# Attention and a mixture on one core: keys scaled where they are copied, and four operations moved to other engines or places

## What is computed

```python
k_sum = k.reshape(B, H, nb, block, D).max(axis=3)
v_sum = v.reshape(B, H, nb, block, D).mean(axis=3)
scores_l = scale * np.matmul(q, k.transpose(0, 1, 3, 2))     # scale = 1 / sqrt(64)
scores_s = scale * np.einsum('bhsd,bhnd->bhsn', q, k_sum) + np.log(block)
scores_l_m = np.where(mask_l, scores_l, -1000000000.0)       # |pos - pos'| < 16
a = softmax(concatenate([scores_l_m, scores_s]))
out = np.matmul(a, np.concatenate([v, v_sum], axis=2))
```

```python
logits = x @ w_gate                       # top 2 of 4, softmax over the two
q, k, v = x @ wq[e], x @ wk[e], x @ wv[e]
ye = causal_softmax(q @ k.T / 8) @ v @ wo[e]
```

## Time and profile before

| | |
|---|---|
| median of 3 runs | 451.85 us (450.61 to 452.22) |
| the profiled execution | 452.24 us, its span 450.4 us |
| TensorE busy | 431.9 us, 96% |
| VectorE, ACT, GpSimd busy | 298.1, 227.6, 134.7 us |
| chain that ended last | PE 85%, DVE 8%, ACT 3%, "issue" 3% |
| DMA | 38.12 MB, mean 85 GB/s |

### The profile page before, as it was taken

The page is one execution under the profiler, slowest core; times in us unless marked ns, Lnnn a source line. Parts: engine busy times, 40 slices in busy tenths (PEclk is TensorE's granted clock), DMA queues, the critical chain, the costliest instruction groups (busy, mean ns, idle before and its releaser), DMA issues.

```text
span 450.4 us, 8603 instructions
## 1 busy us (share of the span) xinstructions
PE 431.9 (96%) x3332; PEld 367.1 (81%) x3332; DVE 298.1 (66%) x549; ACT 227.6 (51%) x591; POOL 134.7 (30%) x170
## 2 busy tenths in 40 slices
PE   8799998998997999999999999999999999999997
PEld 3478996887765789978876899998998898989885
DVE  4794489866467835697666877576675776475453
ACT  6785647766237955677782562434443233233120
POOL 3878583000006412000259056631132022200000
PEclk9989998999999999999999999999999999999999
DMA  8965065000493140000022111122123063201103
GB/s 255 261 190 162 26 179 207 1 2 0 123 287 102 25 142 1 0 1 1 1 95 95 47 48 46 49 93 57 46 87 93 0 235 93 72 24 48 47 2 140
DMA packets 13914, 38.12 MB, mean 85 GB/s; under 512 B 1536, under 2 KB 2480, under 8 KB 13872
## 3 DMA queue, kind: packets, MB, share of 16 engines
q1 hardware_dynamic: 13008, 35.98, 26.2%
q10 hardware_dynamic: 864, 1.57, 0.9%
HBM read 31.99 MB, written 4.72 MB: 81 GB/s over the span
## 4 chain that ended last, share of the span: by engine, by line
PE 85%; DVE 8%; ACT 3%; issue 3%; POOL 0%; ACTq 0%; DVEq 0%; POOLq 0%
PE ps_s L683 34%; PE ps_o L683 19%; PE ps_x L683 14%; PE ps_t L683 10%; PE ps_t L855 4%; PE ps_t L750 2%; ACT PA L1094 2%; DVE nmaxM L1443 1%; DVE nmaxA L1351 1%; PE ps_x L869 1%; DVE QS L1391 0%; DVE PTA L1371 0%; DVE PTM L1454 0%; DVE gate_gt L1423 0%; PE ps_s L936 0%
## 5 line engine op out<-in xcount | busy, mean ns | idle before, releaser
L1331 ACT ACTIVATE HID_h<-HID_raw 128x384 fp32r<-128x384 f32 x48 | 25.1, 525 | 72.3 <-DVE HID_raw L1659 31.3
L632 POOL TENSOR_TENSOR W_raw<-W_raw 128x256 f32<-128x256 f32 x11 | 10.7, 975 | 99.3 <-DMA W_raw<-in_ch 88.6
L1094 ACT ACTIVATE PA<-ps_s,biasA 128x120 f32<-128x120 f32 x96 | 33.7, 381 | 12.7 <-DVE biasA L1355 10.1
L683 PE MATMUL ps_s<-C_h,HID_l 128*128 128x512 f32 x96 | 37.7, 393 | 0.0
L683 PE MATMUL ps_s<-C_l,HID_h 128*128 128x512 f32 x96 | 37.7, 393 | 0.0
L683 PE MATMUL ps_s<-C_h,HID_h 128*128 128x512 f32 x96 | 37.6, 392 | 0.0
L547 POOL TENSOR_TENSOR PA<-PA,denA 128x480 f32<-128x480 f32 x24 | 23.7, 986 | 46.7 <-DVE denA L1364 46.6
L1648 DVE SCALAR_TENSOR_TENSOR HID_l<-HID_raw,HID_h 128x384 fp32r<-128x384 f32 x48 | 28.3, 593 | 10.5 <-ACT HID_h L1331 8.1
L1157 ACT ACTIVATE PM<-ps_s,nmaxM 128x128 f32<-128x128 f32 (+5 forms) x48 | 30.1, 634 | 9.5 <-DVE nmaxM L1443 9.0
L683 PE MATMUL ps_o<-V_h,W_h 128*128 128x384 f32 x96 | 32.8, 342 | 0.1
L683 PE MATMUL ps_o<-V_h,W_l 128*128 128x384 f32 x96 | 32.4, 337 | 0.0
(11 more groups left out here) (255 smaller groups left out, 1269.1 us busy)
## 6 DMA issues: line engine op xcount, KB each, us to landing
W_raw<-in_ch SPq DMA_DIRECT2D x12, 512.0 KB, 3.8
C_raw<-in_ch SPq DMA_DIRECT2D x12, 512.0 KB, 3.8
VW<-in_vw SPq DMA_DIRECT2D x12, 384.0 KB, 9.6
KP<-in_kT SPq DMA_DIRECT2D x8, 384.0 KB, 6.4
VT<-in_vT SPq DMA_DIRECT2D x8, 384.0 KB, 6.4
out_x<-US SPq DMA_DIRECT2D x12, 256.0 KB, 2.0
QT<-in_qT SPq DMA_DIRECT2D x7, 384.0 KB, 7.7
raw<-in_tok SPq DMA_DIRECT2D x4, 384.0 KB, 3.3
```

Source lines behind the costliest of these rows:

```text
L632: pool.tensor_tensor(W[S3], W[A11], W[A21], ALU.subtract).then_inc(w_sum, 1)
L683: return pe.matmul(out, lhsT, rhs, start=start, stop=stop)
L1094: last = act.activation(PA[:, u % NPA, j, :], ps_s[u % 2][:, j % 2, (j // 2) * KC:(j // 2 + 1) * KC], ACT.Exp, bias=biasA[:, u % 4, j:j + ...
L1331: act.activation(*own(s, n, half), ACT.Relu).then_inc(g_hi, 1)
```

## The change

Six things, of which the diff below shows the core.

1. `KW` gets the keys and the maxima times 1/8: ACT's copies take a scale, the other copies become multiplications by a constant (TENSOR_SCALAR on GpSimd and VectorE). The masks and logarithms are no longer raised, the exponentials have no scale, and `nmaxA` is their bias as it is: VectorE's scaling to `biasA` and its semaphore are gone, 24 instructions and as many waits.
2. GpSimd makes the splits of wo and of the first half of tok1 ahead of `no_lows` instead of behind it (N_EARLY = 5), and the last split (second half of tok2) waits for the gate's twelfth step.
3. The six stores of u are issued by SP, behind the loads for batch 1, instead of by ACT; the first means' placing stands between the fourth and the fifth store.
4. In batch 0, TensorE makes the first transposes ahead of the first means, and ACT copies in that order.
5. VectorE's fourth sum of the second weight block stands behind X_l instead of ahead of it.
6. With `biasA` gone, the buffers behind it lie 64 bytes lower.

```diff
+N_EARLY = 5
@@ sync
+            def store_u(b, t):
+                sp.wait_ge(m_u, b * TQ + (t + 1))
+                sp.dma_start(u_d[t * P:(t + 1) * P, :], US1[t][:, :]).then_inc(st_u[t], 16)
...
-                for q in range(2):
-                    place_means(b, q)
+                for t in range(TQ):
+                    if t == TQ - 2:
+                        place_means(b, 0)
+                    store_u(b - 1, t)
+                place_means(b, 1)
@@ gpsimd
-                    pool.tensor_copy(KW[:, r, 4 * i:4 * i + 4, 0:WK], windows(r, 4 * i)).then_inc(a_kwin, 1)
+                    pool.tensor_scalar(KW[:, r, 4 * i:4 * i + 4, 0:WK], windows(r, 4 * i), SCALE, None,
+                                       ALU.mult).then_inc(a_kwin, 1)
...
                 if b == 0:
-                    pool.wait_ge(c_lo, 3)
+                    pool.wait_ge(c_lo, N_EARLY)
...
                 if b == 0:
-                    split(len(PACED))
+                    for n in range(len(PACED), N_EARLY):
+                        split(n)
                 no_lows(b)
                 if b == 0:
-                    for n in range(len(PACED) + 1, N_TOK2):
+                    for n in range(N_EARLY, N_TOK2):
+                        if n == N_TOK2 - 1:
+
+                            pool.wait_ge(m_g, NGATE)
                         split(n)
@@ tensor, sequence
+
+                    if k <= NU + 2:
+                        a_transpose(b, k - 3)
                     if b == 0 and k == 3:
                         a_first_means(b)
-
-                    if k <= NU + 2:
-                        a_transpose(b, k - 3)
@@ scalar
-                                          ACT.Exp, bias=biasA[:, u % 4, j:j + 1], scale=SCALE,
+                                          ACT.Exp, bias=nmaxA[:, u % 4, j:j + 1],
...
-                    act.activation(KW[:, r, 4 * i:4 * i + 4, 0:WK], windows(r, 4 * i), ACT.Copy).then_inc(a_kwin0, 1)
+                    act.activation(KW[:, r, 4 * i:4 * i + 4, 0:WK], windows(r, 4 * i), ACT.Copy,
+                                   scale=SCALE).then_inc(a_kwin0, 1)
...
                 for t in range(TQ):
-                    if more:
-                        store_u(b, t)
@@ vector
-                                      AX.X, ALU.max, negate=True).then_inc(a_mx, 1)
-                    dve.wait_ge(a_mx, b * NU + (u + 1))
-                    dve.tensor_scalar(biasA[:, u % 4, :], nmaxA[:, u % 4, :], SCALE, None, ALU.mult).then_inc(a_max, 1)
+                                      AX.X, ALU.max, negate=True).then_inc(a_max, 1)
...
                 m_x2_lo(b, TQ - 1)
+                if not more:
+                    last_row_sum()
```

More of the change, by code:

```diff
@@ L24 @@
 NEG = -1000000000.0
-RAISE = 1.0 / SCALE
 TQ = S // P
@@ L306, in program @@
         a_zero = sem("a_zero")
-        a_mx = sem("a_mx")
         a_kfill0 = sem("a_kfill0"); a_kfill = sem("a_kfill")
@@ L516, in _ @@
             step(pool.memset(mask_m[0:HALF, :, 0:WK], 0.0))
[L517 to L520 removed]
+            keep(mask_m[0:HALF, :, 0:WK], [[0, 3], [1, WK]], -1, -1, NEG)
+            keep(mask_m[0:HALF, :, 0:WK], [[0, 3], [-1, WK]], 2 * WINDOW - 1, 1, NEG)
+            keep(mask_m[0:HALF, 0, 0:WK], [[1, WK]], -WINDOW, 0, NEG)
+            keep(mask_m[0:HALF, 2, 0:WK], [[-1, WK]], WK - WINDOW - 1, 0, NEG)
             assert steps[0] == N_MASK
@@ L1522, in second_row_sums, with last_row_sum @@
                 dve.tensor_tensor(W[S2], W[S1], W[A11], ALU.subtract).then_inc(w_sum1, 1)
+            def last_row_sum():
+                W = [W_raw[1][:, a, :, :] for a in range(NB7)]
                 dve.wait_ge(w_sum1, 3)
@@ L1623, in _ @@
             dve.memset(KP[:, :, WINDOW + S:PAD_S], 0.0).then_inc(a_zero, 1)
-            fill(mask_m[0:HALF, :, WK:KC], RAISE * LOG0)
+            fill(mask_m[0:HALF, :, WK:KC], LOG0)
             fill(mask_w[:, :], LOG_W)
-            fill(mask_c[:, :], RAISE * LOG_M)
+            fill(mask_c[:, :], LOG_M)
             for r in range(2):
```

18 lines of the change are left out of this document (6 added, 12 removed).

## The result

| | before | changed |
|---|---|---|
| median, us | 451.85 (450.51 to 452.43) | **455.34** (455.07 to 456.21) |
| ratio, 95% interval | | 1.0092 (1.0072 to 1.0112) |
| profiled execution / its span | 452.24 / 450.4 | 455.88 / 454.1 |

I had forecast 447.1, in a range of 445.5 to 449.5. The changed kernel is 3.5 us slower than the one before, and 8.2 us above the forecast.

A forecast was written before the change was run, and what follows sets the result against it. TensorE, busy 431.9 of 450.4 us, was taken as the bound. Terms 2.0 + 1.15 + 0.2 + 0.7 + 0.75 = 4.8 us off the profiled 452.24 gave 447.4, against the median 447.1 us; range 445.5 to 449.5.

The forecast's parts named there:

- the price of the scaled copy: GpSimd's window copies and fills: multiplying by a constant was taken to cost what the plain copy does, 508 ns for 128x384.
- my upper end: GpSimd's scaled copy at the two-input rate: 790 ns, +1.5 us on batch 1's chain, 448.6 us in all; chance 0.12.
- the sign of being wrong that I had named: GpSimd: the prediction is wrong if the scaled copy is above 0.8 us, or VectorE waits for the last split's end.
- The slower rival: GpSimd's scaled copy far dearer, say 1.5 us: batch 1's chain and batch 0's fills late, 454.3 us; chance 0.03.
- Batch 0 hides such a rise: Batch 0's fills: a dearer copy costs nothing there, as they end at 19.84 and TensorE takes the unit at 21.33.
- The gate, 2.0 us: Batch 0's gate: with two GpSimd splits brought forward, VectorE's gate operations are no longer held; 2.0 us won, 1.2 to 2.2.
- the last split takes the gate's place: Batch 0 behind the gate: GpSimd's last split holds VectorE's key remainders, up to 1.9 us lost, 449.0 us; chance 0.07.
- The start of batch 1, 1.15 us at the copy's price: Batch 1 up to unit 6: u stores on SP let unit 2's exponentials and GpSimd's chain start sooner; 1.15 us won.
- The rest of batch 1, 0.2 us: Rest of batch 1's attention: removing the 24 scalings of the maxima, which ACT waited for, wins 0.2 us, 0 to 0.5.
- The end, 0.75 us: End of batch 1's mixture: X_l starts where VectorE's fourth sum did, 0.75 us sooner, 0.5 to 0.8.
- Batch 0's attention, 0.7 us: Batch 0's attention: scaling of the maxima removed and means behind the transposes win 0.7 us, 0 to 1.6.

The follow-up runs named there:

- e9: e5 with GpSimd's copies and fills of batch 0 scaled by one operation instead of two; 449.46 us, ratio 0.9949.
- e1: The changed kernel with GpSimd's window copies and fills made plain copies again, the factor 1/8 left out there; 446.07 us, ratio 0.9898.
- e3: The changed kernel with the scaling of the keys undone (plain copies, masks raised, maxima scaled), all other parts kept; 447.87 us, ratio 0.9927.
- e5: The changed kernel with GpSimd's window copies and fills multiplying by 1/8 and then by 1, two operations in one instruction; 446.13 us, ratio 0.9878.

## Why the prediction was wrong

- **The step that failed** is the price of the scaled copy: "I take the copy's price, as the affine select lies 0.04 us from that", and with it both ends of the bound. The operation took 1.17 us; my upper end was 0.79, and the sign of being wrong that I had named, a scaled copy above 0.8 us, came true. The affine select that I leaned on had 64 partitions, 288 elements and bf16; measured at 384 elements of f32 it takes 0.68 us, not the copy's 0.51. And the arithmetic of a one-input operation is not bounded by that of a two-input one: here the two-input product is the quicker of the two (0.83 against 1.17). The 1.8 cycles an element of the Trainium skill, page "GPSIMD Engine Reference", section "3.1 Elementwise — side-by-side cycle accounting", from which I worked out an estimate of 0.58 us, fit neither the form with one operation (1.17) nor the one with two (0.51); the measurement decides.
- **The slower rival** had the mechanism, with a chance of 0.03 and the reason that "only the row is missing". It also had the size wrong. It set the break-even at 1.25 us a copy; at the 1.17 us found, its own terms (3.6 on the chain in batch 1, 0.1 for the pair of copies at 137.4, 0.2 at the fills of batch 0, less 4.8) would have come out at 451.0, faster than before. The kernel took 455.3. What it left out were the clock behind the long gap (2.06 us) and most of batch 0 (3.3 us by e9).
- **"Batch 0 hides such a rise"** fell. I set the fills' new end against TensorE's arrival at 21.33, but that arrival was late because of the 2.2 us gap, and the gap was 0.6 us this time. The cover was a wait that is not always there; at the price found the fills ended at 21.98, behind my 21.33 too. The four window copies behind them I had not costed at all; what they add is not settled.
- **The gate, 2.0 us**: right. Between the two products that the prediction named it is 11.46 us in the changed kernel for 13.41, 1.95 less, at a granted clock of 1.00. The stretch of my table ends at the next unit's score product, 0.6 to 1.1 us later, and gives 2.41, and 2.56 to 2.58 in e1 and e3. The twelve steps take 2.43 us (61.56 to 63.99), none over 0.26:

```profile
61.56 0.18 DVE L1417 TENSOR_REDUCE gate_max<-VE 128x6 f32<-128x24 f32 x1
...
63.81 0.18 DVE L1435 TENSOR_TENSOR gate_w<-gate_w,gate_s 128x24 f32<-128x24 f32 x1
...
65.17 1.12 DVE L1395 SCALAR_TENSOR_TENSOR KL<-ps_t,KH 64x384 fp32r<-64x384 f32 x2 [1.18 <-ACT KH L1152]
```

  The key remainders beside the last split (64.97 to 66.80 us on GpSimd) keep their 1.12 us, so the rival "the last split takes the gate's place" fell. By the rule of the Trainium skill, page "SBUF — State Buffer", section "Who interferes with whom", a VectorE operation with at most one SBUF input is left alone as long as it doesn't use both ports; for the key remainders the trace agrees.
- **The start of batch 1, 1.15 us at the copy's price**: 1.16 in e5 (7.77 to 6.61). The path through GpSimd's chain, the place and the size were right; with its true price the same chain gave +2.68.
- **The rest of batch 1, 0.2 us**: 0.40 in e5 (13.92 to 13.52), nothing in e3, where the scaling of the maxima stays: so it comes from the removal.
- **The end, 0.75 us**: 0.62 to 0.71. X_l no longer waits behind the fourth sum:

```profile
247.01 0.84 DVE L1528 TENSOR_TENSOR W_raw<-W_raw 128x256 f32<-128x256 f32 x1
247.93 0.69 DVE L1486 TENSOR_TENSOR X_l<-ps_x,X_h 128x512 fp32r<-128x512 f32 x1
248.54 0.88 DVE L1533 TENSOR_TENSOR W_raw<-W_raw 128x256 f32<-128x256 f32 x1
```

- **Batch 0's attention, 0.7 us**: the middle of the eight kernels with quick copies has 62.1 us for the first stretch, 0.65 under before, but their spread of 3.3 us hides a term of this size. The medians leave room for it: e5 is 5.7 us under the kernel before, and its other stretches give 4.6 of that, so by this estimate 1.1 are left for batch 0, give or take 1. It is not settled.

With the copy's price put right, e5, which is the changed kernel in all else, takes 446.13 us, 1.0 under the forecast. So the terms for gate, start and end stood, the rest of batch 1 gave 0.4 for 0.2, the one for batch 0 can't be told from its spread, and the one row that the trace didn't have was worth 9 us.

## What to carry to other kernels

When a change rests on an operation that the trace doesn't show, its price is no number between the nearest rows; give such a change the chance of a real loss, work that loss out through every chain the operation stands in, and measure the operation first in a stretch where its engine is idle. A place counts as covered only if what covers it is work that is always there, not a wait that came about by late loads. And a gap of 5 us on TensorE is to be costed with the slower clock behind it, here 2.1 to 2.7 us.
